# Splitting an expert's weights quarter by quarter behind TensorE, and reading one flag ahead of x, in an attention, routing and maxout kernel

## The reference, cut to what matters

```python
x = attention(q, k, v)                       # 3072 tokens, 512 wide
logits = x @ w_gate + modality_bias[modality_id]
e_idx = np.argmax(logits, axis=1)            # one expert of 8 for each token
...
for e in range(E):
    mask = e_idx == e
    if not mask.any():
        continue
    h = np.maximum(x[mask] @ w1[e], 0.0)     # w1[e]: 512 x 1024
    out[mask] = gate_w[mask, None] * (h @ w2[e])   # w2[e]: 1024 x 512
...
h = np.maximum(np.maximum(x @ w1, x @ w2), x @ w3)  # the maxout layer
return h @ w_out
```

## Time and profile before

| | us |
|---|---|
| three runs, median | 1013.65 |
| three runs, lowest and highest | 1011.21 and 1016.32 |
| the profiled execution, its own time | 1011.33 |
| its span, first to last instruction | 1009.7 |
| PE busy in it | 953.8 |
| DVE busy, ACT busy | 404.0 and 312.7 |
| mean granted TensorE clock | 0.983 |

### The profile page before, as it was taken

How to read it: one execution, slowest core, us unless ns; L and a number is a source line. 1 busy time by engine, 2 the same in 40 slices (tenths; PEclk the granted TensorE clock), 3 DMA queues, 4 the chain that set the end, 5 groups by cost and what they waited for, 6 DMA issues and landing times.

```text
span 1009.7 us, 15521 instructions
## 1 busy us (share of the span) xinstructions
PE 953.8 (94%) x5140; PEld 752.7 (75%) x5140; DVE 404.0 (40%) x1308; ACT 312.7 (31%) x759; POOL 95.4 (9%) x175
## 2 busy tenths in 40 slices
PE   3999999998899999799999839999999999999998
PEld 2777677664478888688888638888888888888887
DVE  5678686875532222532222464312313123123120
ACT  2676767663411111411111333111211211112111
POOL 2112212041200000000000040010100100000000
PEclk9999999998899999899999979999999999999999
DMA  4345655370461111341111031020100200100001
GB/s 102 125 156 182 205 184 196 95 274 12 171 218 42 42 42 48 108 125 42 48 46 42 21 104 42 1 84 1 52 32 0 73 10 0 42 1 11 32 1 42
DMA packets 35955, 76.99 MB, mean 76 GB/s; under 512 B 7488, under 2 KB 9536, under 8 KB 35904
## 3 DMA queue, kind: packets, MB, share of 16 engines
q1 hardware_dynamic: 22016, 49.55, 14.3%
q0 software_dynamic: 6080, 19.93, 6.6%
q10 hardware_dynamic: 7808, 6.87, 2.1%
HBM read 52.74 MB, written 23.59 MB: 76 GB/s over the span
## 4 chain that ended last, share of the span: by engine, by line
PE 69%; DVE 1%; DMA 1%; ACT 1%; issue 0%; POOL 0%; DVEq 0%; ACTq 0%; POOLq 0%
PE bank L651 22%; PE bank L653 22%; PE bank L652 21%; PE bank L678 2%; PE bank L755 1%; PE bank L646 1%; DVE w_lo L1379 0%; POOL yr L487 0%; ACT w_hi L930 0%; DMA yr<-y_sorted,pos_out 0%; DMA y_sorted<-y 0%; DVEq L1397 0%; DVE xT_lo L1401 0%; DVE yT_lo L1497 0%; DVE y L1419 0%
## 5 line engine op out<-in xcount | busy, mean ns | idle before, releaser
L653 PE MATMUL bank<-yT_hi,m_lo 128*128 128x512 f32 x432 | 168.1, 389 | 0.0
L813 ACT ACTIVATE probs<-masked,row_min 128x264 f32<-128x264 f32 (+1 forms) x192 | 93.4, 487 | 80.8 <-DVE row_min L1076 80.1
L651 PE MATMUL bank<-yT_hi,m_hi_b 128*128 128x512 f32 x288 | 112.0, 389 | 0.0
L652 PE MATMUL bank<-yT_lo,m_hi_b 128*128 128x512 f32 x288 | 112.0, 389 | 0.0
L1518 DVE TENSOR_TENSOR b_sb<-bank,a_sb 128x512 f32<-128x512 f32 x36 | 24.9, 692 | 187.9 <-PE bank L653 187.9
L653 PEld LDWEIGHTS bank<-yT_hi,m_lo 128*128 128x128 f32 x432 | 81.1, 188 | 16.8
L1000 ACT ACTIVATE gT_hi<-g_sb 128x512 fp32r<-128x512 f32 x36 | 22.8, 632 | 200.1 <-DVE g_sb L1521 200.1
L651 PE MATMUL bank<-w_hi,xT_hi 128*128 128x512 f32 x192 | 77.3, 403 | 6.2 <-DVE w_lo L1379 5.0
L1076 DVE CUSTOM_DVE_ANT_0 masked<-bank,masks 128x264 f32<-128x264 f32 (+1 forms) x192 | 70.5, 405 | 27.9 <-PE bank L509 26.8
L651 PE MATMUL bank<-w_hi,hT_hi 128*128 128x512 f32 x192 | 76.7, 400 | 5.1 <-DVE w_lo L1379 5.1
L509 PE MATMUL bank<-kT,qT 64*128 64x264 f32 (+2 forms) x384 | 67.2, 429 | 12.6 <-issue 11.3
(11 more groups left out here) (209 smaller groups left out, 1590.0 us busy)
## 6 DMA issues: line engine op xcount, KB each, us to landing
w_sb<-in_moe_w SPq DMA_DIRECT2D x6, 2048.0 KB, 10.5
xr<-x_sorted POOLq DMA_DIRECT2D x28, 256.0 KB, 3.0
y_sorted<-y ACTq DMA_DIRECT2D x26, 256.0 KB, 2.0
kT<-in_k_t SPq DMA_DIRECT2D x16, 400.0 KB, 4.4
qT<-in_q_t SPq DMA_DIRECT2D x16, 384.0 KB, 3.3
v_in<-in_v_p SPq DMA_DIRECT2D x16, 384.0 KB, 3.0
out<-o_sb SPq DMA_DIRECT2D x24, 256.0 KB, 2.0
m_sb<-in_moe_w SPq DMA_DIRECT2D x6, 768.0 KB
```

The costliest lines, as they stand in the source:

```text
L651: pe.matmul(psum, a_hi, b_hi, start=first, stop=False)
L652: pe.matmul(psum, a_hi, b_lo, start=False, stop=False)
L653: return pe.matmul(psum, a_lo, b_hi, start=False, stop=last)
L813: last = act.activation(probs[n % 2][:, hd, 0:win_of(t)], masked[n % 2][:, hd, 0:win_of(t)], ACT.Exp, bias=row_min[:, n % 2, hd:hd + 1], s ...
```

## The change

ACT's wait for the whole previous tile becomes a wait for a quarter of it: two new semaphores, `w1_used` and `w2_used`, are raised by PE after each of the first three quarters of every `up` and `down`, and ACT waits for them ahead of quarters 0, 1 and 2; ahead of quarter 3 it still waits for `up_done` or `down_done`. DVE loses its own wait for the previous tile; it waits for ACT's high parts. On both engines one flag is read at the start of an iteration in place of three, the other two where they are used. `split_w1(2i + 1)` moves ahead of `keep_xT(i, 1)`, which is now called inside it: behind the first quarter when there is a new expert, and behind the raising of the counters when there is not.

```diff
+        w1_used, w2_used = sem("w1_used"), sem("w2_used")
...
             def up(i, par):
                 for c in range(KC):
...
                         if c == KC - 1:
                             mm.then_inc(up_done, 1)
+                    if c < KC - 1:
+                        mm.then_inc(w1_used, 1)
...
             def down(i, par, out_bank):
...
+                    if f % 2 == 1 and f < FC - 1:
+                        mm.then_inc(w2_used, 1)
                 mm.then_inc(down_done, 1)
...
+            pe.sem_inc(w1_used, 3 * 2)
+            pe.sem_inc(w2_used, 3 * 2)
...
-            def split_hi(j, flag, dst, src, loaded, done, value, made, chunks):
+            def split_hi(j, flag, dst, src, loaded, used, done, value, made, chunks, between=None):
                 with act.If(flag > 0):
                     act.wait_ge(loaded, flag)
-                    act.wait_ge(done, value)
                     for c in range(4):
                         at = slice(c * chunks // 4, (c + 1) * chunks // 4)
+                        if c < 3:
+                            act.wait_ge(used, 3 * (j - 1) + c + 1)
+                        else:
+                            act.wait_ge(done, value)
                         act.activation(dst[:, at, :], src[:, at, :], ACT.Copy).then_inc(made, 1)
+                        if between and c == 0:
+                            between()
                 with act.If(flag < 1):
                     act.wait_ge(made, 4 * j)
                     act.sem_inc(made, 4)
+                    if between:
+                        between()
...
-                    flags = [first_of(2 * i + n) for n in range(3)]
-                    keep_xT(i, 1)
-                    split_w1(2 * i + 1, flags[1])
-                    split_w2(2 * i, flags[0])
+                    flag_1 = first_of(2 * i + 1)
+                    split_w1(2 * i + 1, flag_1, lambda: keep_xT(i, 1))
+                    split_w2(2 * i, first_of(2 * i))
...
                     keep_xT(i + 1, 0)
-                    split_w1(2 * i + 2, flags[2])
-                    split_w2(2 * i + 1, flags[1])
+                    split_w1(2 * i + 2, first_of(2 * i + 2))
+                    split_w2(2 * i + 1, flag_1)
...
             def split_lo(...):
                 with dve.If(flag > 0):
                     dve.wait_ge(loaded, flag)
-                    dve.wait_ge(done, value)
                     for c in range(4):
                         dve.wait_ge(hi_made, 4 * j + c + 1)
                         dve.tensor_tensor(dst, src, hi, ALU.subtract).then_inc(made, 1)
+                        if between and c == 0:
+                            between()
```

More of the change, by code:

```diff
@@ L934, in split_hi, with split_w1 @@
                     act.sem_inc(made, 4)
-            def split_w1(j, flag):
-                split_hi(j, flag, w1_hi, w1_sb, w1_loaded, up_done, 2 * j + 1, w1_hi_made, KC)
+                    if between:
+                        between()
+            def split_w1(j, flag, between=None):
+                split_hi(j, flag, w1_hi, w1_sb, w1_loaded, w1_used, up_done, 2 * j + 1, w1_hi_made, KC, between)
             def split_w2(j, flag):
-                split_hi(j, flag, w2_hi, w2_sb, w2_loaded, down_done, j + 1, w2_hi_made, FC)
+                split_hi(j, flag, w2_hi, w2_sb, w2_loaded, w2_used, down_done, j + 1, w2_hi_made, FC)
             def first_of(j):
@@ L1369, in _, with split_lo @@
             nt = dve.value_load(n_tiles[0:1, 0:1], min_val=1, max_val=TMAX)
-            def split_lo(j, flag, dst, src, hi, loaded, done, value, hi_made, made, split, chunks):
+            def split_lo(j, flag, dst, src, hi, loaded, hi_made, made, split, chunks, between=None):
                 with dve.If(flag > 0):
                     dve.wait_ge(loaded, flag)
-                    dve.wait_ge(done, value)
                     for c in range(4):
@@ L1387, in split_lo, with split_w1 @@
                     dve.sem_inc(made, 4)
-            def split_w1(j, flag):
-                split_lo(j, flag, w1_lo, w1_sb, w1_hi, w1_loaded, up_done, 2 * j + 1, w1_hi_made, w1_lo_made, w1_split, KC)
+                    if between:
+                        between()
+            def split_w1(j, flag, between=None):
+                split_lo(j, flag, w1_lo, w1_sb, w1_hi, w1_loaded, w1_hi_made, w1_lo_made, w1_split, KC, between)
             def split_w2(j, flag):
-                split_lo(j, flag, w2_lo, w2_sb, w2_hi, w2_loaded, down_done, j + 1, w2_hi_made, w2_lo_made, w2_split, FC)
+                split_lo(j, flag, w2_lo, w2_sb, w2_hi, w2_loaded, w2_hi_made, w2_lo_made, w2_split, FC)
             def first_of(j):
```

## The result

The changed kernel takes 999.63 us (median of four runs, 996.38 to 1000.68). The kernel before takes 1013.89 us (median of four, 1011.21 to 1016.32). The ratio is 0.9849, with a 95% interval of 0.9829 to 0.9868. The profiled execution took 996.38 us, with a span of 994.7 and a mean granted clock of 0.990.

The account below looks back on a forecast made before the run. PE bounds the kernel, so time is won only where it stands still or runs at the lower clock. 8.41 + 5.54 + 1.08 - 0.6 = 14.4 us gained, from 1013.65 to 999.2 us; range 995 to 1004.5.

Parts of the forecast that it names:

- What bounds the kernel, and the marker: PE bounds the span; by DVE's copy of the last y, the two changes of expert cost 8.41 and 5.54 us.
- w1 at a change: At a new expert's w1, about 0.3 us of waiting stays of 2.50, for x and not weights.
- w2 at a change: At a new expert's w2, ACT decides the first quarter's start and nothing stays of the 2.56 us wait.
- The clock: Lower PE clock at the first change of expert: 2.87 us, 1.4 each behind two of four equal pauses.
- The first iteration: DVE's chain to `xT_lo` drops two reads and adds the step over the split: 1.08 us gained, 0.27 waiting left.
- What costs nothing: In the other iterations the moved reads, PE's increments and the split step are covered; x is kept 0.6 us sooner.
- The sum: Whole kernel: 8.41 + 5.54 + 1.08 - 0.6 = 14.4 us gained, giving 999.2 us from the median 1013.65.
- The partial gain: Rival: ACT or DVE late at the w1 split, or half clock elsewhere; gain 9.7 us, thus 1004; chance 0.2.
- The early split: Rival denied it: `w1_used` short until the tile's end, only the reads won, 1.08 us, 1012.6; chance 0.04.
- Slower: Rival: a split step of 3.5 us delays x, PE losing 1.8 us in each of 11 iterations; 1019; chance 0.02.

Follow-up runs that it names:

- w2 only: The kernel before, with the quarter-by-quarter waits for w2 alone: 1007.04 us, ratio 0.9924 to the kernel before.
- the reads behind x: The kernel before, whole-tile waits kept, with the flags read after `keep_xT(i, 1)` instead of before it: 1009.22 us, ratio 0.9981.
- the order only: The changed kernel, but ACT waits for the whole old tile ahead of the first quarter: 1016.14 us, ratio 1.0016 to the kernel before.
- the quarters and the old order: The changed kernel, with all flags read first and the second tile's x kept ahead of the w1 split: 1000.42 us, ratio 0.9863.
- three flags: The changed kernel, with all flags read at the start of an iteration on both engines: 1003.45 us, ratio 0.9888 to the kernel before.

## Why the prediction was right

Forecast 999.2 us, measured 999.63; forecast gain 14.4, measured 1013.89 - 999.63 = 14.3. The changed kernel's two further sets of runs give 1010.4 - 996.31 = 14.1 and 1010.54 - 996.68 = 13.9. By its own steps:

**What bounds the kernel, and the marker.** Right. The excess of 8.41 and 5.54 us became 0.33 each; the two iterations gave 13.35 where 8.41 + 5.54 - 0.6 = 13.35 was forecast.

**w1 at a change.** Right within 0.1 us at each step. Counted from the first matmul of `up(i, 0)` (400.18 after, 401.55 in the earlier trace rows): the first high part at 2.88 (forecast 2.90), the low part at 3.97 (3.98), `xT_lo` at 5.11 (5.15), PE at 6.14 (6.19). The new wait, for x, is 0.21 us, with 0.3 forecast. Without the new order it is 0.86 and for weights; without the quarters it is 3.30.

The first of these fits has luck in it. From the end of y's store ACT takes 403.06 - 401.59 = 1.47 us to the first high part, and took 405.54 - 402.96 = 2.58 to `xT_hi`, so 1.11 less; 1.5 - 0.4 = 1.1 was forecast. But the two reads were worth 1.22. On ACT's sequencer the three reads begin at 403.36, 404.24 and 404.85 and end at 405.46: the first takes 0.88 us, with a load of 0.55, and each other 0.61, and it is the first that stays. Entering the split costs 0.1 more than going to `xT_hi` did, not 0.4. Reads put 0.3 too high and the entry put 0.3 too high cancel.

**w2 at a change.** Right that nothing stays, wrong in the reason. I had ACT decide the start of the first quarter, because it reads a flag (0.75) and steps over the w1 split (0.4) behind `xT_hi`. It is PE at all four quarters: ACT stands idle for PE 0.57 us ahead of the first high part and 0.30 ahead of each other, at PE's own pitch of 1.36 us. The read costs nothing here. ACT's sequencer does it from 414.27 on, while the engine is still at `hT_hi` and at `xT_hi` (414.44 to 415.07):

```profile
L958 ACTq TENSOR_LOAD <-tab_i x1: 291/291/291, 414.4 to 414.4; - x1
```

In these traces a read has a price only where the engine has run dry, as at the start of an iteration. Here it changes nothing, since either way there is over 1 us to spare.

**The clock.** The term was 2.87 us, from two of four pauses. The runs bear it out as a thing that follows the pauses. At changes of expert the clock fell behind 11 of 14 pauses of 2.5 to 3.3 us (2 of 4 before, 2 of 2 with w2 only, 3 of 4 with the reads behind x, 4 of 4 with the order only), behind 4 of 4 of 3.6 to 3.7 us, and behind none of 1.3 us or less. One fall costs 1.4 to 1.6 us after the shorter and 2.1 on average after the longer ones. A long pause isn't sure to bring it: in the first iteration the clock fell during the pause of 3.63 us with w2 only, and stayed at 1.00 behind that of 3.66 with the quarters and the old order. The wait for the loop's first x, 2.7 to 4.1 us in all fourteen profiles, had the lower clock in or behind it in twelve. What I left open, whether something else made the first change differ from the second, has its answer: equal pauses end differently from place to place, at either change. The Trainium skill ("TensorE: Matmul & The Clock Gate", Part 1, the HAM clock gate) has the monitor behind the gate run free of the kernel; by that rule, too, no change of expert is the safe one, and the traces agree with 11 of 14. At 11 in 14 the kernel before would lose 4 x 0.79 x 1.5 = 4.7 us rather than 2.87 on average, an estimate from these rows. The run times don't bear it out: it would make the gain some 16 us, and the three pairs of medians give 13.9 to 14.3. So 2.87, taken from one execution with two falls of four, is a term that happened to fit; how often the kernel before loses the clock is not known from one profile.

**The first iteration.** Mis-sized by a little: 1.08 us on DVE's chain forecast, 0.91 measured. A read costs DVE 0.72 (forecast 0.74), the step over the split 0.54 (forecast 0.4, from the branches alone). PE's wait fell by 0.19 only, and 0.27 of it was forecast to be left where 1.01 is; but that wait is no measure of the gain. `up(1, 1)` starts when DVE lets it, so how early PE comes doesn't count, and its start moved by the whole 1.34 us (285.04 to 283.70), of which 0.91 are the change's.

**What costs nothing.** Right for the changed kernel: ordinary iterations last 24.46 us as before, so the increments on PE, the moved reads and the step have their cover. In the second iteration `xT_lo` starts 306.33 - 302.54 = 3.79 us behind the copy of y, where it was 308.34 - 303.89 = 4.45, so 0.66 sooner (forecast 0.6). The run with three flags shows how thin that cover is.

**The sum.** In the trace the change gave 13.35 + 0.91 = 14.26 us, with 14.43 forecast. The spans differ by 15.0, because 0.43 came from the clock ahead of the loop and 0.3 from the maxout layer. That the run medians differ by 14.3 as well is partly luck: the forecast carried the median's 2.3 us over the profiled execution along unchanged, and in the changed kernel the median lies 3.25 over it. Parts that the change doesn't touch move by more than that error. From the last y to the end the span takes 422.1 to 422.7 us in nine of the fourteen profiles of this document and 423.9 to 424.4 in the other five, and the changed kernel has both, 422.4, 422.5 and 424.4.

**The rivals.** The partial gain needed a wait of over 1 us or a lost clock behind the same work; there was neither. The early split did come. "Slower" turned on a step of 3.5 us, which takes 0.54 on DVE.

## What to carry to other kernels

Where one engine rewrites a buffer that another reads in pieces, let it wait for the pieces: here that took four idle stretches of 2.5 us and the lower clock behind most of them. Look then at the order around the new work, since whatever stands behind that work (x here) becomes the next wait, and every register read or branch that is moved ahead of it is paid in each iteration as soon as the cover is thinner than it. When a step is moved, follow its semaphores as well: fourteen small index steps were free to move, but the load that they released was not.

## What the runs showed of the hardware

Where DVE has nothing queued, the read of one flag into a register costs it 0.72 us in all (2.17 for three). On ACT the first of three reads takes 0.88 us and each other 0.61, though the loads are shown with 0.55 and 0.28. Stepping over an `If` and through its other arm costs DVE 0.54 us, though its branches are shown with 0.05. Such work shows in the timeline only as a gap ahead of the next instruction, and not even as that where the sequencer does it while the engine is still busy, as at 414.27 us.

Pauses of PE of 2.5 us were enough for the lower clock in most cases (11 of 14 from 2.5 to 3.3 us), and 0.86 and 1.27 us, twice each, were not. DVE and ACT made the new weights while PE ran, and PE's matmuls kept their pitch of 0.23 us (414.53 to 424.74).

A load of 2 MB issued beside three transfers of x of 256 KB each took their median landing from 3.1 to 6.6 us.
